# Work of a delta-rule layer's first chunks reordered over four engines ahead of two mixture layers

## The reference, cut to what matters

```python
# 4 batches x 8 heads, 768 times, head size 48
k_n = k / (norm(k) + 1e-6)
for t in range(768):
    y[t] = q[t] @ state
    state += beta[t] * outer(k_n[t], v[t] - k_n[t] @ state)
x = y, with the heads side by side            # 3072 tokens x 384
h = x @ w_in; x = act1(h) @ w_out             # 2048 hidden, act1 piecewise: 0, (h+1)^2/4, h
h = x @ w_in2; out = max(h, 0)**2 @ w_out2
```

## Time and profile before

| | us |
|---|---|
| median of three runs (998.6 to 1000.44) | 1000.19 |
| the profiled execution, its own time | 1000.15 |
| its span, first to last instruction | 998.2 |
| PE busy | 981.7 (98%) |
| DVE busy | 583.1 (58%) |
| ACT busy | 419.2 (42%) |
| POOL busy | 25.4 (3%) |

### The profile page before, as it was taken

The page is one execution under the profiler, slowest core; times in us unless marked ns, Lnnn a source line. Parts: engine busy times, 40 slices in busy tenths (PEclk is TensorE's granted clock), DMA queues, the critical chain, the costliest instruction groups (busy, mean ns, idle before and its releaser), DMA issues.

```text
span 998.2 us, 24906 instructions
## 1 busy us (share of the span) xinstructions
PE 981.7 (98%) x10566; PEld 804.3 (81%) x10566; DVE 583.1 (58%) x1465; ACT 419.2 (42%) x749; POOL 25.4 (3%) x34
## 2 busy tenths in 40 slices
PE   6899999999999999999999999999999999999998
PEld 6578788888888888888888888888888888888887
DVE  7769878776877687769535774433434334334332
ACT  4777544433434434424445553333333233333332
POOL 2510000000000000000000000000000000000000
PEclk9889999999999999999999999999999999999999
DMA  6342232003200410020003411001010010000000
GB/s 217 97 160 72 69 97 77 10 18 94 76 10 18 114 56 18 18 65 33 2 12 128 158 64 64 1 1 64 0 64 1 1 64 1 27 6 1 32 1 32
DMA packets 28413, 50.97 MB, mean 51 GB/s; under 512 B 2320, under 2 KB 15760, under 8 KB 28304
## 3 DMA queue, kind: packets, MB, share of 16 engines
q1 hardware_dynamic: 28304, 49.39, 15.3%
HBM read 39.94 MB, written 9.44 MB: 49 GB/s over the span
## 4 chain that ended last, share of the span: by engine, by line
PE 96%; ACT 2%; issue 1%; DMA 1%; DVE 0%; SPq 0%; DVEq 0%; ACTq 0%
PE psum L1120 40%; PE psum L1096 39%; PE psum L903 3%; PE psum L880 2%; PE psum L972 2%; PE psum L920 2%; PE psum L856 1%; PE psum L1009 1%; PE psum L929 1%; PE psum L1017 1%; PE psum L1040 1%; PE psum L1004 1%; ACT ring L622 1%; PE psum L1013 0%; DMA kt_sb<-in_k_t 0%
## 5 line engine op out<-in xcount | busy, mean ns | idle before, releaser
L1120 PE MATMUL psum<-g_hi,w 128*128 128x512 f32 x1152 | 392.1, 395 | 0.1
L1096 PE MATMUL psum<-x_hi,w 128*128 128x512 f32 x1152 | 387.0, 390 | 0.0
L1382 DVE TENSOR_TENSOR g_lo<-act_g,g_hi 128x512 fp32r<-128x512 f32 x192 | 132.6, 691 | 214.5 <-ACT g_hi L746 214.3
L1120 PEld LDWEIGHTS psum<-g_hi,w 128*128 128x128 f32 x1152 | 216.1, 188 | 50.8 <-issue 2.0
L1096 PEld LDWEIGHTS psum<-x_hi,w 128*128 128x128 f32 x1152 | 216.2, 188 | 45.6 <-issue 0.2
L746 ACT ACTIVATE g_hi<-act_g 128x512 fp32r<-128x512 f32 x192 | 121.4, 632 | 273.3 <-PE psum L1120 239.4
L1120 PE MATMUL psum<-g_lo,w 128*128 128x512 f32 x576 | 224.6, 390 | 0.0
L1096 PE MATMUL psum<-x_lo,w 128*128 128x512 f32 x576 | 224.1, 389 | 0.0
L1376 DVE TENSOR_TENSOR act_g<-act_g 128x512 f32<-128x512 f32 x96 | 66.4, 692 | 112.9 <-ACT act_g L739 112.9
L1096 PEld LDWEIGHTS psum<-x_lo,w 128*128 128x128 f32 x576 | 108.1, 188 | 22.4 <-issue 0.2
L1120 PEld LDWEIGHTS psum<-g_lo,w 128*128 128x128 f32 x576 | 108.2, 188 | 20.6
(11 more groups left out here) (101 smaller groups left out, 607.5 us busy)
## 6 DMA issues: line engine op xcount, KB each, us to landing
kt_sb<-in_k_t SPq DMA_DIRECT2D x24, 256.0 KB, 4.0
qt_sb<-in_q_t SPq DMA_DIRECT2D x24, 256.0 KB, 3.6
kn_sb<-in_k_n SPq DMA_DIRECT2D x20, 256.0 KB, 4.1
ring<-in_v_s SPq DMA_DIRECT2D x24, 192.0 KB, 2.7
between_layers<-y_out SPq DMA_DIRECT2D x6, 768.0 KB, 5.1
x_sb<-between_layers SPq DMA_DIRECT2D x6, 768.0 KB, 5.7
result<-y_out SPq DMA_DIRECT2D x5, 768.0 KB, 3.9
wi_st<-in_w_in SPq DMA_DIRECT2D x7, 384.0 KB, 3.1
```

What stands on the lines that cost most here:

```text
L1096: ins = pe.matmul(h_ps[n % 2][:, :], w_in_part(layer, f // GW, part)[:, kt, fs], x[:, kt, :], start=(kt == 0 and j == 0), stop=(kt == KT - ...
L1120: ins = pe.matmul(acc[kt][:, :], w_out_part(layer, f // GW, part)[:, f % GW, ds], g[n % 2][:, :], start=(f == 0 and j == 0), stop=(f == NF ...
L1382: dve.tensor_tensor(g_lo[n % 2][:, :], act_g[n % 2][:, :], g_hi[n % 2][:, :].bitcast(F32), ALU.subtract).then_inc(g_lo_ready, 1)
```

## The change

It has these parts.

- The four grams of chunk 1 (`gram_of(4)` to `gram_of(7)`) move on PE from behind the outputs of chunk 0 and from steps 0 to 2 to a place right behind the keys by queries. They go to tensors of their own, `gram1`, which lie where the last group of first-layer weights comes later.
- On ACT the splits of weight groups 0 and 1 and the scaling of v are spread between earlier copies, the copies of the four grams follow, and the split of group 3 comes before chunk 0's chain (it was in steps 0 and 1). The scaling of v for row block 3 moves to DVE (`scaled_values_first`).
- On DVE chunk 1's inverse starts ahead of `x_low_first`, with three of its 31 steps (`AHEAD`); the pieces of the steps are cut anew.
- POOL makes the low part of group 3 too, which DVE made, and clears `x_inv` ahead of the low parts of group 1.
- Of the twelve unread products of 256 columns in chunk 0's inverse the first six go. In the chain the one of 256 columns per row block becomes one of 384 and one of 128 between the two halves, and one of 128 is added ahead of the first product.

```diff
@@ def stage(stack, name):
-        weights = [[first_layer.enter_context(nc.sbuf_tensor(f"w1_{g}", [P, 2, 2, GW * DM], F32R)) for g in range(NG)]]
+        weights = [[first_layer.enter_context(nc.sbuf_tensor(f"w1_{g}", [P, 2, 2, GW * DM], F32R)) for g in range(NG - 1)]]
+        ahead_of_last = ExitStack()
+        gram1 = [ahead_of_last.enter_context(nc.sbuf_tensor(f"gram1_{b}", [P, H, LATE], F32)) for b in range(B)]
+        ahead_of_last.close()
+        weights[0].append(first_layer.enter_context(nc.sbuf_tensor(f"w1_{NG - 1}", [P, 2, 2, GW * DM], F32R)))
@@ def staged(layer, g):
+        def gram_at_chunk(n):
+
+            return gram1 if n == 1 else gram
+
+        def hi_turn(layer, g):
+
+            return layer * NG + g if layer or g not in (2, 3) else 5 - g
+
@@ def g_ps(m):
-            return (bank[6], bank[7]) if m == B else (bank[5], bank[7])
+            if m < 2 * B:
+                return ((bank[4], bank[5]), (bank[6], bank[7]), (bank[2], bank[3]))[m % B % (B - 1)]
+            return bank[5], bank[7]
@@ def gd_ps(n, hp):
+        scaled_last = sem("scaled_last")
...
-        FIRST_PIECES = (0, 2, 4, 6, 8, 10, 12, 13, 15, 16, 18, 19, 21, 23, 25, 27, 29, BLK - 1)
...
+        BY_POOL = EARLY + 1
+        AHEAD = 3
+        FIRST_PIECES = (AHEAD, 5, 7, 9, 11, 12, 14, 15, 17, 18, 20, 21, 23, 25, 26, 28, 29, BLK - 1)
@@ def gram_at(t, f):
-            at = ({0: 1, 1: 2, 2: 3}, {4: 1, 5: 2, 6: 3}, {5: 2, 6: 3})[min(t, 2)]
+            at = ({}, {4: 1, 5: 2, 6: 3}, {5: 2, 6: 3})[min(t, 2)]
@@ def split_at(n):
-            if t == 0 and f // 3 + EARLY < NG and f % 3 < 2:
+            if t == 0 and BY_POOL <= f // 3 + EARLY < NG and f % 3 < 2:
@@ def load_weights(layer, g, w_in, w_out):
-                    split = 2 * (g + 1 - (1 if at == 2 else 2) + layer * NG)
+                    split = 2 * (hi_turn(layer, g - 1 if at == 2 else g - 2) + 1)
...
-                    if g == 2 and not layer:
-                        sp.wait_ge(w_lo_early, split)
+                    if layer or g > BY_POOL:
+                        sp.wait_ge(w_lo_ready, 2 * (layer * NG + (g if at == 2 else g - 1) - BY_POOL))
...
-                        sp.wait_ge(w_lo_ready, split - 2 * EARLY)
+                        sp.wait_ge(w_lo_early, 2 * (g if at == 2 else g - 1))
@@ def low_parts(g):
-                    pool.wait_ge(w_hi_ready, 2 * g + out_part + 1)
+                    pool.wait_ge(w_hi_ready, 2 * hi_turn(0, g) + out_part + 1)
...
-            low_parts(1)
...
-            low_parts(2)
+            for g in range(1, BY_POOL):
+                low_parts(g)
@@ def gram_out(m):
-                if m >= B:
+                if m >= 2 * B:
...
-                    wait(act, s_done, B * NB * (m // B - 1))
+                if m >= 3 * B:
+                    act.wait_ge(s_done, B * NB * (m // B - 1))
...
-                    act.activation(gram[m % B][0:LATE, hp * HP:(hp + 1) * HP, :], blocks, ACT.Copy).then_inc(gram_ready, 1)
+                    act.activation(gram_at_chunk(m // B)[m % B][0:LATE, hp * HP:(hp + 1) * HP, :], blocks, ACT.Copy).then_inc(gram_ready, 1)
@@ def split_weights(layer, g, out_part):
+                if not layer and g == NG - 1:
+                    act.wait_ge(s_done, B * NB)
@@ def square_part(n):
-                        act.wait_ge(w_lo_early, 2 * EARLY)
+                        act.wait_ge(w_lo_early, 2 * (EARLY - 1))
@@ def drain(layer, t):
-                act.wait_ge(w_lo_ready, 2 * (NG - EARLY))
+                act.wait_ge(w_lo_early, 2 * BY_POOL)
+                act.wait_ge(w_lo_ready, 2 * (NG - BY_POOL))
@@ def second_step(n):
-            gd_out(1, 1)
-            for m in range(B):
-                kq_out(m)
...
+            scaled_first(0, 0, H)
+            gd_out(1, 1)
...
-            for k in range(NB):
-                scaled_first(k, 0, H)
+            kq_out(0)
+            kq_out(1)
+            scaled_first(1, 0, H)
+            kq_out(2)
+            kq_out(3)
+            for m in range(B, 2 * B):
+                gram_out(m)
+            scaled_first(2, 0, H)
+            split_weights(0, EARLY, 0)
+            split_weights(0, EARLY, 1)
...
-            gram_out(B)
@@ def diagonals_of(n, hp):
+                    pe.wait_ge(x_lo_ready, B)
@@ def gram_of(m):
-                elif n == 1 and b == 0:
-                    pe.wait_ge(first_u_act, OWN * HALVES * NB)
-                    pe.wait_ge(first_u_dve, (B - OWN) * HALVES * NB)
-                elif n == 1 and b == 1:
-                    pe.wait_ge(x_lo_ready, B)
+                elif n == 1 and b < B - 1:
+                    pe.wait_ge(kq_plain, 2 * (b + 2))
+                elif n == 1:
@@ def substitute(k):
-                                            gram[b][0:i * BLK, place(0, j), (i - 1) * BLK:i * BLK],
+                                            gram_at_chunk(n)[b][0:i * BLK, place(0, j), (i - 1) * BLK:i * BLK],
@@ def first_solve(k, part):
-                    pe.wait_ge(kq_plain, 2 * (B - 1))
-                pe.wait_ge(scaled0, H * k + (part + 1) * HH)
+                    pe.wait_ge(gram_ready, 2 * B + 4)
+                if k < NB - 1:
+                    pe.wait_ge(scaled0, H * k + (part + 1) * HH)
@@ def low_parts_ready(layer, g, out_part):
-                if at > 2 * EARLY:
-                    pe.wait_ge(w_lo_ready, at - 2 * EARLY)
+                if at > 2 * BY_POOL:
+                    pe.wait_ge(w_lo_ready, at - 2 * BY_POOL)
@@ def first_product(n):
-                    pe.wait_ge(w_hi_ready, 2 * (layer * NG + f // GW) + 1)
+                    pe.wait_ge(w_hi_ready, 2 * hi_turn(layer, f // GW) + 1)
@@ def second_product(n):
-                    pe.wait_ge(w_hi_ready, 2 * (layer * NG + f // GW) + 2)
+                    pe.wait_ge(w_hi_ready, 2 * hi_turn(layer, f // GW) + 2)
...
+            for m in range(B, 2 * B):
+                gram_of(m)
...
-            for j in range(19, BLK - 1):
+            for j in range(25, BLK - 1):
...
-                keep_busy(2 * P, bank[0])
-                for part in range(HALVES):
-                    first_substitute(k, part)
+                keep_busy(3 * P, bank[0])
+                first_substitute(k, 0)
+                keep_busy(P, bank[0])
+                first_substitute(k, 1)
...
-            gram_of(B)
...
+            keep_busy(P, bank[1])
@@ def gains_turn(n):
-                    dve.wait_ge(scaled0, NB * H)
+                    dve.wait_ge(scaled0, (NB - 1) * H)
+                    dve.wait_ge(scaled_last, 1)
@@ def residual(k):
+            def scaled_values_first(k):
+
+                dve.wait_ge(v_loaded[k], 16)
+                dve.wait_ge(norm_turned, 1)
+                values = ring[:, k, :, :].rearrange("p (a h) e -> p a h e", h=2)
+                by = norm_t[:, 0, k * H:(k + 1) * H].rearrange("p (h a) -> p a h", h=2).unsqueeze(3).to_broadcast([P, HP, 2, D])
+                dve.tensor_tensor(values, values, by, ALU.mult).then_inc(scaled_last, 1)
+
@@ def residual_first(k, part):
-                dve.wait_ge(scaled0, H * k + (part + 1) * HH)
+                if k < NB - 1:
+                    dve.wait_ge(scaled0, H * k + (part + 1) * HH)
+                else:
+                    dve.wait_ge(scaled_last, 1)
@@ def second_step(n):
+            scaled_values_first(NB - 1)
...
+            start_inverse(1)
+            inverse_steps(1, 0, AHEAD)
...
-            start_inverse(1)
```

## The result

| | us |
|---|---|
| median after (1003.68 to 1005.61, 5 runs) | 1004.49 |
| median before in the same comparison (998.6 to 1000.61, 5 runs) | 1000.19 |
| ratio, 95% interval | 1.0048 [1.0033, 1.0062] |
| the profiled execution of after, its own time and its span | 1005.18, 1003.5 |

The change makes the kernel 4.3 us slower, where 5.8 us faster was forecast. The first rival, VectorE held at the port it shares with GpSimd, had 1001.5 for four waits and 1003.3 for five.

A forecast was written before the change was run, and what follows sets the result against it. PE, busy 981.7 of 998.2 us, was taken as the bound, with gains only in the first 107 us. Terms -4.85 - 2.55 + 1.6 = -5.8 us took 1000.15 to 994.3 us; range 991.0 to 1000.5.

The forecast's parts named there:

- The first rival: Ahead of x_lo: the port holds DVE every time; 1001.5 us with four waits, 1003.3 with five; chance 20%.
- row blocks: Chunk 0's chain: ScalarE's copies start earlier, -1.2 us; the clock holds in blocks 2 and 3, -1.3 us.
- outputs: End of chunk 0's chain: all four at full clock take 3.5 us instead of 5.32, -1.8 us.
- outputs to the first product, with the port: Ahead of the mixture: 1.35 us needed instead of 1.90, -0.55 us; one wait of DVE for POOL, +1.6 us.
- first product to step 9 (the grams): Steps 0 to 2: three grams of chunk 1 leave PE's full stretch, -2.55 us.
- the port: DVE's early inverse beside POOL's low parts: one wait of 1.8 us less 0.2 us to spare, +1.6 us.
- The longer unread products: Row blocks: 512 unread columns for 256 lie in ScalarE's copy time, charged nothing; 0.7 us a block at most.
- The rival of the fallen clock: Row blocks: the clock falls all the same, block 3 takes 5.2 us, total 998.1 us; chance 13%.
- one for one: From about 107 us on: PE is full and passes on all that is gained before.
- The low parts of group 3: Moved from DVE to POOL: ready at about 59 us, needed by PE at step 6, some 80 us, so hidden.

The follow-up runs named there:

- e2: The changed kernel, but POOL starts the low parts of weight groups 2 and 3 only once the low parts of x are done; 1001.10 us.
- e3: The changed kernel, but the low parts of weight group 3 are made by DVE in steps 0 and 1, as before; 1001.38 us.
- e4: The kernel before, with chunk 1's inverse begun (three steps) ahead of x_lo and x_inv cleared ahead of group 1's low parts; 1002.66 us.
- e9: The changed kernel, with POOL clearing (memset, reads nothing) the low parts of weight groups 2 and 3 instead of subtracting; 999.13 us.
- e1: The changed kernel, with the low parts of x ahead of the start of chunk 1's inverse on DVE again; 999.96 us.
- e13: e12 with chunk 1's gains on DVE moved behind the last row block's residual; 994.72 us, ratio to before 0.9956.
- e15: e13 with the load of weight group 2 held until the third row block is solved; 995.89 us.
- e5: The changed kernel with DVE's order and POOL's share of before; early grams, ScalarE order and longer unread products kept; 1000.17 us.
- e7: e6 with POOL's clear of x_inv back behind group 1's low parts; 998.80 us, ratio to before 1.0001.
- e12: e8 with step 8's residual ahead of g_lo and three steps of chunk 1's inverse right behind x_lo; 997.48 us.
- e8: e7 with the unread products of before in the row blocks (256 columns, none between the halves); 998.55 us.
- e6: e5 with the transfers of k_n for items 2 and 3 issued ahead of the load of weight group 4; 1000.73 us.

## Why the prediction was wrong

The terms of the forecast against the profiles of before and after (spans 998.2 and 1003.5), in us:

| stretch | forecast | measured |
|---|---|---|
| row blocks, 38.16 to 51.92 before | -1.2 - 1.3 = -2.5 | +1.3 |
| outputs | -1.8 | -1.7 |
| outputs to the first product, with the port | -0.55 + 1.6 = +1.05 | +5.4 |
| first product to step 9 (the grams) | -2.55 | 0.0 |
| the rest of the span | 0 | +0.3 |
| sum | -5.8 | +5.3 |

**The step that failed first is the port: +1.6 for one wait.** There were four ahead of `x_lo`, 6.4 us together, and a fifth in the chain. The forecast took one wait, since it had seen a single row, 358 ns for 209, and argued that POOL "would have to win against a DVE that always has one ready". It does not have to win a race. It has its next instruction ready too. In after, e2, e3 and e4 one of DVE's instructions got through for each one of POOL's, at 1.8 us a turn: e4, e3 and after give two, two and four waits ahead of `x_lo` for two, two and four low parts of POOL, and e9 gives none where POOL reads nothing. That the two take turns is not a rule, though: in e1 one instruction of DVE stood through two of POOL's (3.33 us). The 358 ns look like the tail of such a wait, by where DVE's instruction came in POOL's 1.8 us (POOL ended at 49.10, the row at 49.15). Of the four `x_lo` that the forecast names as free of it, only the first two ran beside POOL, which had ended at 58.1 us; e1, where all four did, bears the reading out. The page SBUF — State Buffer of the Trainium skill, section Who interferes with whom, makes the lock exclusive and whole for the instruction, and the waits of 1.5 to 1.7 us beside instructions of 1.8 agree. The forecast quoted it and gave the rival 20%.

**The rival's price came near, in part by luck.** It had 1001.5 to 1003.3 for 1004.5 measured. It counted the four waits ahead of `x_lo` rightly, but its fifth, in the chain, cost PE nothing in after; its half clock cost more than the 1.7 us that it had (from the first product to the first state change behind it 7.04 us, in e13 4.26); and it had no loss in the row blocks.

**The row blocks (-1.2 - 1.3) failed second.** ScalarE was in time, copies from 38.04 us (forecast 37.9), and the clock held in the first two blocks. But two pauses (0.71 and 1.84) stood where one of 1.09 was kept, and the clock fell behind the longer one, so that the third block took 5.34 us for 3.4. Together the blocks took 3.8 us more than forecast. The length of these pauses is the open cause here; no semaphore explains them, and e15 does not settle it. In the experiments another loss stands in the same place: the residual of the last block behind the `dn` that POOL held, for which PE waited 0.7 to 2.2 us in e1, e2, e3, e5 and e7 to e12. The terms can be had: in e13's profile, with the gains out of the way, short pauses and a clock that held, the blocks took 3.44, 3.88 and 3.56 us. One reading of the forecast was off, too: in the first block of before PE was idle for 1.8 of the 2.3 us from 38.9 to 41.2, not for about half.

**The longer unread products** were charged at nothing. In time e7 and e8 show no difference that can be told (0.25 us in the median), and e8's clock did not fall where they were short. But where the clock does fall they cost: in after's third block they took 1.65 + 0.80 = 2.45 us, where before has 1.22. The rival of the fallen clock had this right, 5.2 us for the 5.34 of that block.

**The outputs (-1.8)** were right in size: 3.63 us for 3.5, in after and in e13. In after that is in part luck: the clock did not hold from 38 to 60 us, as forecast, but fell and rose again 0.2 us ahead of the outputs. In e1 and e9 it was still 0.50 in most of them.

**The grams (-2.55)** are off PE's full stretch, as forecast, but the sentence that what is gained ahead of 107 us is passed on "one for one" was wrong. Behind the grams lay two more gates: `k_n` at step 3, which no wait of before showed (2.5 us in e5), and DVE at step 9, whose wait of 1.1 us was said to stay and grew (2.0 to 2.2 in e6 to e8). In e13, with the first opened and the second eased, the stretch from the first product to step 9 is 99.31 - 55.57 = 43.74 us for 45.43: 1.7 of the 2.55 arrive. In after itself `k_n` was not waited for, since everything came late, and step 9 waited 1.3 us; there the half clock behind the wait for `x_lo` took the grams' gain.

**The low parts of group 3** on POOL were called hidden for PE, and are, but they are two of the four waits.
